# Row sums of an attention softmax applied to its output instead of its probabilities, on one core

## The reference, cut to what matters

```
scores = scale * q @ k^T                      # scale = 1/8
scores = where(bucket(q) == bucket(k), scores, -1e9)
scores = scores - max(scores, axis=-1)
attn   = exp(scores)
attn   = attn / (sum(attn, axis=-1) + 1e-9)
out    = attn @ v
x      = out as (1536, 512)
x      = ((x @ w1) * (x @ w2)) @ w3 @ w_out
x      = (sigmoid(x @ w_gate) * (x @ w_val)) @ w_out2
```

## Time and profile before

| | |
|---|---|
| Time, 3 runs | median 761.7 us (758.96 to 762.28) |
| The profiled execution | 763.15 us, its span 761.4 us |
| Granted TensorE clock, mean | 0.996 |
| TensorE matmuls busy | 735.6 us (97%) |
| VectorE busy | 466.0 us (61%) |
| ScalarE busy | 465.4 us (61%) |
| GpSimd busy | 358.0 us (47%) |

### The profile page before, as it was taken

The page is one execution under the profiler, slowest core; times in us unless marked ns, Lnnn a source line. Parts: engine busy times, 40 slices in busy tenths (PEclk is TensorE's granted clock), DMA queues, the critical chain, the costliest instruction groups (busy, mean ns, idle before and its releaser), DMA issues.

```text
span 761.4 us, 12753 instructions
## 1 busy us (share of the span) xinstructions
PE 735.6 (97%) x4136; PEld 674.0 (89%) x4136; DVE 466.0 (61%) x1015; ACT 465.4 (61%) x857; POOL 358.0 (47%) x299
## 2 busy tenths in 40 slices
PE   6799999999999998899999999999999999999998
PEld 4588888889787787899999999999999999988886
DVE  5789999999999898544144635532333335764000
ACT  5789999999998987633537225645345354705100
POOL 3867374653739599444646400235635644240000
PEclk9899999999999999999999999999999999999999
DMA  5682644527273300110010000001100010501001
GB/s 148 222 186 62 164 106 116 151 70 195 82 182 77 91 29 0 50 35 29 31 51 28 1 1 1 26 31 29 51 32 28 31 52 0 166 1 69 28 28 41
DMA packets 26609, 51.80 MB, mean 68 GB/s; under 512 B 4160, under 2 KB 12688, under 8 KB 26576
## 3 DMA queue, kind: packets, MB, share of 16 engines
q1 hardware_dynamic: 26272, 51.32, 24.7%
q10 hardware_dynamic: 304, 0.07, 0.0%
HBM read 29.43 MB, written 3.15 MB: 43 GB/s over the span
## 4 chain that ended last, share of the span: by engine, by line
PE 72%; DVE 10%; issue 6%; ACT 5%; SPq 2%; DMA 2%; POOL 1%; DVEq 0%; ACTq 0%; POOLq 0%
PE pair_bank L1328 14%; PE pair_bank L1330 14%; PE pair_bank L1329 14%; PE bank L1330 6%; PE bank L1329 6%; PE bank L1328 6%; PE bank L1241 4%; PE pair_bank L1229 4%; PE bank L1256 3%; DVE rowmax L943 3%; DVE pt_lo L976 3%; ACT prob L670 2%; DMA sq<-q_codes 1%; ACT pt_hi L630 1%; PE bank L1290 1%
## 5 line engine op out<-in xcount | busy, mean ns | idle before, releaser
L1094 DVE TENSOR_TENSOR u<-bank,u 128x384 f32<-128x384 f32 x80 | 44.4, 556 | 136.5 <-ACT u L630 126.8
L630 ACT ACTIVATE u<-pair_bank 128x384 f32<-128x384 f32 x120 | 58.6, 491 | 106.9 <-PE pair_bank L1330 106.8
L976 DVE TENSOR_TENSOR pt_lo<-bank,pt_hi 128x384 fp32r<-128x384 f32 x192 | 97.5, 549 | 6.6 <-ACT pt_hi L630 6.3
L670 ACT ACTIVATE prob<-pair_bank,ebias,escale 128x768 f32<-128x768 f32 x96 | 95.3, 992 | 6.0 <-DVE ebias L954 6.0
L1229 PE MATMUL pair_bank<-mk,sq 128*128 128x384 f32 x384 | 92.3, 363 | 6.1 <-ACT prob L670 1.9
L630 ACT ACTIVATE pt_hi<-bank 128x384 fp32r<-128x384 f32 x192 | 85.0, 491 | 18.0 <-PE bank L1241 15.5
L943 DVE TENSOR_REDUCE rowmax<-pair_bank 128x1 f32<-128x768 f32 x96 | 91.0, 948 | 5.1 <-PE pair_bank L1229 5.1
L1241 PEld LDWEIGHTS bank<-ident,prob 128*128 128x128 f32 x576 | 65.2, 141 | 28.8 <-DVE pt_lo L976 13.1
L1241 PE MATMUL bank<-ident,prob 128*128 128x128 f32 x576 | 84.4, 280 | 6.5 <-ACT prob L713 2.8
L1328 PE MATMUL pair_bank<-y_hi,g_hi 128*128 128x384 f32 x240 | 80.3, 335 | 0.0
L1229 PEld LDWEIGHTS pair_bank<-mk,sq 128*128 128x128 f32 x384 | 62.8, 191 | 16.4 <-issue 10.3
(11 more groups left out here) (165 smaller groups left out, 1976.5 us busy)
## 6 DMA issues: line engine op xcount, KB each, us to landing
sq<-hl SPq DMA_DIRECT2D x45, 192.0 KB
mk<-hl SPq DMA_DIRECT2D x15, 384.0 KB
qk_raw<-in_qk SPq DMA_DIRECT2D x7, 768.0 KB, 5.5
w_raw<-in_w SPq DMA_DIRECT2D x16, 256.0 KB, 2.7
v_raw<-in_v SPq DMA_DIRECT2D x16, 192.0 KB, 2.7
wo_raw<-in_wo SPq DMA_DIRECT2D x12, 256.0 KB, 3.7
out<-out_sb SPq DMA_DIRECT2D x12, 256.0 KB, 2.0
mk<-hl SPq DMA_DIRECT2D x15, 192.0 KB
```

The source lines that it names most:

```text
L630: return act.activation(dst, src, ACT.Copy)
L670: act.activation(prob[k % 3][:, :].rearrange("p (c n) -> p c n", c=KC), pair_bank[k % 2][:, :, 0:HALF], ACT.Exp, bias=ebias[:, k:k + 1], s ...
L976: dve.tensor_tensor(pt_lo[(k // UQ) % 2][cut], t_bank[j][:, 0:384].rearrange("p (t n) -> p t n", t=3), pt_hi[(k // UQ) % 2][cut].bitcast(F ...
```

## The change

1. In pairs 0 to 6 the probabilities are no longer multiplied by the inverse row sum. The transposes wait for the exponential alone. The twelve inverses of a pair are made by two additions and one reciprocal in step 0 of the next pair, turned by a 32x32 transpose, written to DRAM in four transfers, and read back by two transfers that spread each head's 768 inverses over 64 partitions (`inverse_all`). GpSimd multiplies the pair's output by them (`attention_scale`). Pair 7 multiplies the probabilities as before.
2. The bias and scale of the exponential are made by one instruction from the negated maximum. For that the factor 1/8 moves into q: GpSimd multiplies the raw q by it in place (two operations for a pair) before it is rounded, and rounds k first. In pair 0 ScalarE and VectorE apply it in the splits.
3. In the SyncE queue the four writes stand between the loads of w3 and v and the load of q and k; the two spreading reads stand between the load of q and k and the first head's nine transfers. One pair more is written out ahead of the loops.

```
 def qk_split(p):                                  # GpSimd
-    pieces = [(t, half) for t in range(2) for hf in range(2)]
-    for t, cols in pieces:
+    pieces = [(t, half) for t in (1, 0) for hf in range(2)]
+    for n, (t, cols) in enumerate(pieces):
+        if n == 2:
+            pool.wait_ge(bits_done, p + 1)
+            for _, half in pieces[2:]:
+                pool.tensor_tensor(one(qk_raw[:, 0, half]), one(qk_raw[:, 0, half]),
+                                   scale.broadcast_to([128, 1, HALF]), ALU.mult).then_inc(q_scaled, 1)
+        if t == 0:
+            pool.wait_ge(q_scaled, 2 * p - 3 + n)
         rounded(one(hl[:, 2 * t, cols]), one(qk_raw[:, t, cols])).then_inc(qk_hi_done, 1)
+def attention_scale(p):                           # GpSimd, last in pair p
+    pool.wait_ge(inverses_spread, 32 * p)
+    pool.wait_ge(x_added, 2 * p)
+    pool.tensor_tensor(x_f[:, p - 1, :], x_f[:, p - 1, :], one(inverse_all), ALU.mult).then_inc(x_done, 2)
...
 def pair(p, first=False, last=False):             # SyncE
     load_w3(p + 1, 0, p + 1)
     load_v(p + 1, 0, p + 1)
+    if not first:
+        write_rows(p)      # wait inverses_turned; 4 transfers of [12 x 32] to inverse_rows in DRAM
     if not last:
         load_qk(p + 2, 4 * p + 5, p + 2)
+    if not first:
+        spread_rows(p)     # wait rows_written, x_done; 2 transfers, DRAM -> 64 partitions x 768 each
     assemble(0, p + 2, STEPS * p + QT)
...
-dve.tensor_reduce(rowmax[:, k:k + 1], pair_bank[k % 2], AX.XY, ALU.max)
-dve.tensor_scalar(escale[:, k:k + 1], rowmax[:, k:k + 1], -PEN / 2, SCALE, ALU.is_gt, ALU.mult)
-dve.tensor_scalar(ebias[:, k:k + 1], rowmax[:, k:k + 1], escale[:, k:k + 1], -1.0, ALU.mult, ALU.mult)
+dve.tensor_reduce(neg_max[:, k, 0:1], pair_bank[k % 2], AX.XY, ALU.max, negate=True)
+dve.scalar_tensor_tensor(exp_in[:, k, :], neg_max[:, k, 0:1].broadcast_to([128, 2]),
+                         PEN / 2, neg_max[:, k, :], ALU.is_lt, ALU.mult)
...
+def sums_eps_of(p, hd):  dve.tensor_scalar(sums_eps[:, 6 cols], rowsum[:, 6 cols], 1e-9, None, ALU.add)
+def inverse_of(p):       dve.reciprocal(inverses[:, 0:STEPS], sums_eps[:, :])
+def turn(p):             dve.transpose(inverses_t[:, :], inverses[:, :])
...
 def transpose(p, k, last):                        # TensorE
-    pe.wait_ge(norm_done[k % UQ], 4 * p + k // UQ + 1)
+    if last: pe.wait_ge(norm_done[k % UQ], k // UQ + 1)
+    else:    pe.wait_ge(exp_done, s + 1)
```

More of the change, by code:

```diff
@@ L368, in assemble, with write_rows, spread_rows, pair @@
                 assemble_q_codes(hd)
-            def pair(p, last=False):
+            def write_rows(p):
+                if not isinstance(p, int):
+                    sp.compute_val(32 * (p - 1))
+                sp.wait_ge(inverses_turned, p)
+                at_least(sp, inverses_spread, 32 * (p - 1))
+                for b in range(0, 128, 32):
+                    sp.dma_start(inverse_rows[:, b:b + 32], inverses_t[b:b + STEPS, :]).then_inc(rows_written, 16)
+            def spread_rows(p):
+                if not isinstance(p, int):
+                    sp.compute_val(64 * p)
+                    sp.compute_val(2 * (p - 1))
+                sp.wait_ge(rows_written, 64 * p)
+                at_least(sp, x_done, 2 * (p - 1))
+                for hd in range(2):
+                    sp.dma_start(inverse_all[D * hd:D * hd + D, :].rearrange("p (k n) -> p k n", k=QT),
+                                 inverse_rows[QT * hd:QT * hd + QT, :].partition_broadcast(D)).then_inc(
+                                     inverses_spread, 16)
+            def pair(p, first=False, last=False):
                 load_w3(p + 1, 0, p + 1)
                 load_v(p + 1, 0, p + 1)
+                if not first:
+                    write_rows(p)
                 if not last:
                     load_qk(p + 2, 4 * p + 5, p + 2)
+                if not first:
+                    spread_rows(p)
                 assemble(0, p + 2, STEPS * p + QT)
@@ L404, in _ @@
             load_v(0, 1, 0)
-            pair(0)
-            with sp.Fori(1, PAIRS - 2) as p:
+            pair(0, first=True)
+            pair(1)
+            with sp.Fori(2, PAIRS - 2) as p:
                 pair(p)
@@ L553, in pair @@
                     v_split(p, 1)
+                    attention_scale(p)
                 if ahead:
@@ L1032, in pair @@
                         row_max(*nxt)
-                    sum_eps(p, k)
+                    if last:
+                        sum_eps(p, k)
                     if nxt:
[L1035 to L1039, removed]
+                        exp_inputs(*nxt)
+                    if last:
+                        inverse(p, k)
+                    if last and k not in NORM_ON_ACT:
                         normalise(p, k)
+                    if k == 0 and not first:
+                        sums_eps_of(p - 1, 1)
                     if k > 0:
@@ L1043, in pair @@
                     elif not first:
+                        inverse_of(p - 1)
                         transposed_lo(p - 1, STEPS - 1)
+                        turn(p - 1)
+                    if k == QT and not last:
+                        sums_eps_of(p, 0)
                     if k == 2 and not last:
@@ L1067, in _ @@
             row_max(0, 0)
-            exp_scale(0, 0)
-            exp_bias(0, 0)
+            exp_inputs(0, 0)
             pair(0, first=True)
-            with dve.Fori(1, PAIRS - 1) as p:
+            pair(1)
+            with dve.Fori(2, PAIRS - 1) as p:
                 pair(p)
@@ L1318, in pair @@
                         values(p, u4, part)
-                    transpose(p, k)
+                    transpose(p, k, last)
             def keep_warm(count):
```

103 lines of the change are left out of this document (69 added, 34 removed).

## The result

The changed kernel takes 777.9 us (median of 4 runs, 774.63 to 778.76) against 761.7 us: 1.0205 times as long, 95% interval 1.017 to 1.0241. The forecast of 758 us had the wrong sign, and its range of 751 to 766 us missed.

A forecast was written before the change was run, and what follows sets the result against it. TensorE was taken to bound middle pairs now, the operands' loop after the change. Pair 0 +1.5, five cycles -3.0, pair 6 -2.3 and pair 7 0.0 sum to -3.8, giving a median of 758 us, range 751 to 766.

The forecast's parts named there:

- one small operation: VectorE's bias and scale instruction in each step, counted within about 2.1 us of VectorE work left per step.
- pair 7: Last pair: -0.4 us for one small VectorE operation less, +0.4 for 2 us more on GpSimd; sum 0.0.
- The road of the operands: Loading the next pair's operands: landing 2.6 us later, TensorE waiting 0.7 to 0.9, cycle 32.8 us, five cycles -3.0.
- Rival 3: Slow spreading reads ahead of the nine transfers make operands 5.6 us late: +10.2, 772 us; chance 0.14.
- TensorE's own cycle: Middle pair with TensorE as the bound: 31.3 us of work plus 0.6 of waits, 31.9 us.
- The landing of pair 1's operands: End of pair 0: operands that landed at 49.6 come later, with the scores of pair 1 at 51.1.
- GpSimd's wait for the reads: In `attention_scale`, behind L439: this wait and the multiplication come before work not needed until the next pair, so free.
- pair 6: No load of q and k, GpSimd decides: done at 250.4, ScalarE waits 1.4 us, -2.3 (bounds -4, 0).
- Pair 0: First pair: its savings are lost and pair 1's operands land later, +1.5 us (bounds +0.5, +2.2).
- rival 1: Spread hidden and TensorE the bound in middle pairs, cycle 31.9 us: -8.3, 753.4 us; chance 0.23.
- a sign of being wrong as a whole: Time moving behind 310 us, where the prediction counted nothing.
- The fixed cost of 2 us: About 2 us per DMA transfer, so 4 and more for the round trip through DRAM; the sum stayed the same.

The follow-up runs named there:

- e3: The changed kernel with bias and scale of the exponential made by two one-operand instructions in pair 7 alone; 776.18 us.
- e8: The changed kernel with the fill and value product ahead of the waiting scores of pair 1 in step 10 of pair 0; 778.25 us.
- e2: The kernel before with only the fused bias and scale instruction added, the factor 1/8 of the scores left out; 783.12 us.
- e12: The changed kernel without GpSimd's multiplications of q, the factor 1/8 left out, the fused instruction kept; 770.53 us.
- e4: The kernel before with only the inverse sums applied to the output; two instructions for bias and scale, q untouched; 752.44 us.
- e1: The changed kernel with bias and scale made by two instructions again, q still scaled on GpSimd; 768.18 us.
- e6: e1 with the two spreading reads behind the first head's nine transfers instead of ahead of them; 771.88 us.
- e10: The kernel before with only the factor 1/8 moved into q on GpSimd; 766.97 us.
- e11: e4 with the fused instruction, its second tensor in PSUM, the row maximum not subtracted; 755.28 us.
- e7: e4 with GpSimd's last multiplication of the output moved behind the preparation of the next stage in pair 7; 754.82 us.
- e9: e7 with the TensorE order of e8 in step 10 of pair 0; 751.17 us.
- e5: The changed kernel, fused instruction kept, its second tensor in PSUM, so that the row maximum is not subtracted; 767.85 us.

## Why the prediction was wrong, step by step

- **The failed step is the price of the added instruction.** The prediction counts it among what is left on VectorE as "one small operation", and takes 0.4 us off pair 7 for it. It takes up to 1.76 us (3.38 in e3 and e8), stands between the maximum and the exponential in each of 96 steps, and costs +22 us by itself (e2). In a middle pair it is +2.0 us (34.0 in e12 against 32.05 in e4). In pair 7 it is +6.9 us (40.5 against 33.6 of e1), not -0.4. The rows held the warning: the earlier trace rows show a VectorE instruction of 2.11 us beside a GpSimd one, and the prediction drew on that only for what is removed. It didn't ask whether what is added is of a kind that can be held too.
- **The road of the operands was the right second loop, and its term was too small.** Forecast: waits of 0.7 to 0.9 us in step 10 and pairs of 32.8. Measured without the hold (e1): waits of 0.75 to 2.30, mean 1.5, pairs of 33.1 to 34.7; the five cycles give +2.2 us (169.17 against 166.96) where -3.0 stood. e4 and e6 show the two contributors: without the two multiplications one wait of 0.6 is left, with the reads moved back four of five pairs are 32.1 to 33.1. Rival 3, slow reads, was not it: in e4 the reads stand in the same place and the pairs are 32.05.
- **TensorE's own cycle was right**: forecast 31.9, measured 32.05 (e4). (VectorE's part of a step is 2.2 us by the page before, 0.95 + 0.15 + 2 x 0.55, and not 2.1; two small operations stand there in e4 instead of one.) The landing of pair 1's operands was forecast for 51.1 and measured at 51.5, in part by luck: the multiplications move the issue of the last small transfer from 41.72 to 42.98 (44.57 in e10), but its way to the landing alone differs by some 5 us between executions without them, 8.54 us in e11 and at most 3.5 in e4. Right were also the free writes, GpSimd's wait for the reads, which costs e4's middle pairs nothing though it is 18.7 us long, and pair 6 (forecast -2.3, e1 -2.0: 28.80 us between the marks against 30.80; ScalarE waits 1.54 us there for GpSimd's sums, forecast 1.4). Its sum has a slip: 248.4 + 1.6 + 1.97 - 1.3 is 250.7 and not 250.4, which would have made the forecast -2.0.
- **Pair 0 was sized at +1.5 and is +5.2.** Of this 2.0 are the landing, 2.4 the clock behind the long wait, which had no term, and 0.8 the steps behind it.
- **Pair 7 without the hold of L1010** is +1.2 (33.6 against 32.38), inside the bound of +2. The prediction gave GpSimd's last multiplication as the reason; e7 and e9 have it in the same late place and take 31.9 and 33.25 us. What goes with the longer pair 7 is one VectorE multiplication of 2.3 us instead of 0.62.
- With the hold taken out, the sum by these sizes is +4.5 + 2.2 - 2.0 + 1.2 = +5.9 in the span (e1: 767.3 against 761.4). So the two multiplications alone would have spoilt the forecast too: a faster kernel comes from part 1 alone (752.4, near the 753.4 of rival 1 with its cycle of 31.9), and part 2 costs 25.4 us on top of it. What the prediction named as a sign of being wrong as a whole, a move behind 310 us, did not come.
- **The fixed cost of 2 us**, which the prediction takes from the section "Anatomy of one DMA" of the Trainium skill, stands there for transfers that GpSimd issues. This kernel's come from SyncE, and no term of the sum used it. Here each of the two reads took 3.2 to 6.0 us from issue to landing.

Open: why the last small transfer of pair 0 takes 6.7 to 8.5 us in the other traces in which it was followed (before, after, e1, e5, e10, e11, e12) and at most 3.5 in e4's, and what decides whether a held instruction meets one GpSimd operation or four in a row. Nine shorter transfers, or the factor 1/8 on an engine with room, were not tried.

## What to carry to other kernels

Before an added instruction is counted as small, look at which memory each of its tensors comes from and at who runs beside it; columns say nothing of a hold. Where a loop has slack, take from the slack both what is added on it and what the other loop gets shorter by, and look for the queue that a new read joins. And run a bundled change in its parts: here one part gives 0.9% (e4), and the other costs more than that.

## What the runs showed of the hardware

A VectorE instruction on 128x2 elements with two SBUF tensors takes 0.15 us alone and 1.14 us beside a GpSimd operation of 1.29; where four GpSimd operations follow each other it takes up to 3.38 us (e3, e8). GpSimd's own operations are not longer for it (L474 on 128x384, pairs 0 to 6: 826 ns in the mean; the same in e1, without such an instruction: 828). Beside VectorE's multiplication of 128x768 they can be: 2.26 us where VectorE's takes 0.62 (e7), 1.86 where it takes 2.31 (e9).

TensorE's granted clock was 0.54 for 5.9 us behind a wait of 3.7 us and 0.51 behind one of 4.48 (e1). Behind shorter waits both are found: it stayed at 1.00 behind waits of 1.09 and 2.06 (e10) and 2.30 us (e1), and fell behind one of 2.26 in e5:

```profile
155.30:158.50 3.20, 3.20 (x9) 2.91 (x10) 1.11 (x2) 0.00 (x0) 0.00 (x0) 0.50 0.99 223
```

So the length of the wait alone does not tell. That pair of e5 takes 35.65 us where those with waits of 1.62 to 1.84 us and the full clock take 33.5 to 33.65.
